# Row chunks of every fourth feature in the x blocks, and weight slices loaded by GpSimd, in a fused attention and expert kernel

## The chip, the cores and the metric

The kernel runs on one core of a Trainium2 chip. The metric is the device time of one execution in microseconds (us); lower is better. Where several executions are compared, the median is taken.

## What is computed

Three stages follow each other: attention over a window of 128 positions and four sink positions, a top-1 mixture of experts, and a feed-forward layer with a squared ReLU. All is float32. The change is in the third stage alone.

```python
def reference(**kwargs):
    attn_out = _attn_ref(**attn_kwargs)              # 4 x 8 heads, 768 positions, 64 wide
    x = attn_out.transpose(0, 2, 1, 3).reshape(3072, 512)
    x = _moe_ref(x=x, **moe_kwargs)                  # x + gate * relu(x @ w1[e]) @ w2[e], skipped rows keep x
    return _moe2_ref(x=x, **moe2_kwargs)

def _moe2_ref(x, w_in, w_out):                       # 3072 x 512, 512 x 2048, 2048 x 512
    h = x @ w_in
    r = np.maximum(h, 0.0)
    g = r * r
    return (g @ w_out).astype(np.float32)
```

## The kernel before

The first two stages leave x as rows of 512 floats in a DRAM tensor, x_rows. In the third stage each matrix product is made from two rounded parts, an upper and a lower one (upper = a copy to the rounded type by ScalarE, lower = source minus upper by VectorE), with three matmuls for one: lower weights by upper data, upper by upper, upper weights by lower data.

Both matrix products of the third stage use a Strassen-like form: the operands are split in 2 x 2 blocks, and seven products of blocks replace eight. The products are numbered 1 to 7; TensorE takes them in the order 1, 5, 6, 2, 7, 4, 3 (in step 0: 1, 2, 5, 6, 7, 4, 3). A product of the first layer is 12 matmuls of 128x512. Products 1 and 2 use plain blocks of x, products 5, 6, 7 and 4 use differences of blocks (`x_sum`), product 3 a plain one.

The first layer has three chunks of 1024 tokens (m), each with four steps that differ in the weight slice (s); so there are 12 steps t = 4m + s. In a step ScalarE copies product 1 from PSUM to q1 (`p1_copy`, line 1086) and makes block 11 (`block11`, lines 1092 and 1094), VectorE makes the three other blocks (`u2` line 1919, `u3_z22` lines 1925 and 1930, `z21` line 1941, `z12` line 1947) and squares them (line 1935), and SyncE stores four results of 512 KB in g_rows (`store_g`, line 629). The next step's `p1_copy` waits until the store of q1 has landed; product 5 waits for `z12` of the step before; product 3 waits for `u3_z22`, which follows product 7. The second layer then has three chunks of seven products of four units, 12 matmuls each (`unit`, lines 1514, 1515 and 1519), which read g_rows back; a unit's parts are made at lines 1110 and 1956.

The x blocks. SyncE loads x for chunk 1 in step 2 and for chunk 2 in step 5, in `load_x` (line 592): 8 blocks of 512 tokens by 128 features, each by four loads of 32 partitions. A run in DRAM is 32 floats, 128 bytes. VectorE turns each block in squares of 32 (`turn_later`, line 1900), two of the eight turns in step 2 and six in step 3 for chunk 1, four in step 5 and four in step 6 for chunk 2. For the second half of chunk 0 the same is done in the opening (`first_in`, `turn_first`, line 1893); the first half is turned by TensorE (line 1528). The x blocks overlie the buffer of the weight slices, so they can't be loaded while it is used.

The weight slices. Slices s = 0 and 1 of the first layer's weights are ready when it begins. `later_w` holds six more: k = 0 and 1 are slices s = 2 and 3 of the first layer, k = 2 to 5 the four slices of the second layer. Slice k is loaded into `w_in8` by two loads of 512 KB that SyncE issues (lines 584 and 585), GpSimd makes four sums of it (lines 864 to 869), ScalarE three upper parts (`slice_upper`, line 1080) and VectorE three lower parts (`slice_lower`, line 1912; semaphore s_wpl). SyncE issues them in the order of its queue: slice 0 before the opening, slice 1 in step 1, slice 2 at the begin of step 9 after the stores of step 8, slices 3 and 4 at the begin of steps 10 and 11, slice 5 in step 11. The parts of slices 2, 3 and 4 are made in steps 9, 10 and 11: on ScalarE behind `p1_copy`, on VectorE behind `u2`. All queues are in order; the order is written out by hand.

The last results of the second layer are turned by VectorE (line 1982) and stored by SyncE in `store_y` (line 668), four stores of 32 partitions for each half.

## Time and profile before

| | |
|---|---|
| time, median of 3 runs | 920.34 us (919.03 to 921.26) |
| time of the profiled execution | 921.18 us |
| its span in the profile | 919.5 us |
| TensorE busy | 853.1 us, 93% of the span |
| VectorE busy | 680.8 us, 74% |
| ScalarE busy | 454.9 us, 49% |
| GpSimd busy | 121.5 us, 13% |
| DMA moved | 155.34 MB, 99869 of 142678 packets under 512 bytes |

In the rows, PE is TensorE's matmuls, PEld its weight loads, DVE VectorE, ACT ScalarE, POOL GpSimd, SP SyncE; SPq is SyncE's queue. L1478 is line 1478 of the kernel. Times are in us from the start of the span unless they are marked otherwise. "x16" counts instructions. In a timeline the brackets hold the idle time of the engine before the instruction and what ended it. Neighbouring matmuls overlap in the timeline: from start to start a 128x512 one takes 0.227 us at the full clock. The granted clock is a share of full speed, 2.4 GHz. "DMA to landing" is the time from issue until the data is there.

### The profile page before, as it was taken

Reading aid. Unit: us, or ns where it says so; the run is one execution under the profiler, and the core shown is the slowest. Engines: PE = TensorE matmul, PEld = TensorE weight load, DVE = VectorE, ACT = ScalarE, POOL = GpSimd, SP = SyncE. Lnnn points to the kernel's source line nnn. Section 1 sums busy time; section 2 is a strip of 40 time slices with the busy share of each in tenths; the row PEclk is TensorE's granted clock in tenths of the full one; section 3 lists DMA queues with packets and bytes.
Section 4 is the critical chain, followed back from the end, with each engine's and each line's share of the span. In section 5 each row is a group of like instructions: output and inputs, shape, how many; then the busy total and the mean of one; then the engine's idle time right before and its main releaser. Section 6 shows DMA issues by size and latency. Waiting matters only on the chain.

```text
span 919.5 us, 16261 instructions
## 1 busy us (share of the span) xinstructions
PE 853.1 (93%) x4960; PEld 690.0 (75%) x4961; DVE 680.8 (74%) x1533; ACT 454.9 (49%) x900; POOL 121.5 (13%) x170
## 2 busy tenths in 40 slices
PE   9999999999999999969959999977869999999996
PEld 7778777767888887748837878766657888888885
DVE  5787899876777769667748578754479779868964
ACT  7888999855666668332214113222233434334341
POOL 3112222233211123110200000022220000000000
PEclk9999999999999999989979999989979999999999
DMA  5556665187566686332462553322474683576433
GB/s 200 173 165 211 229 224 174 70 287 272 202 225 238 246 289 227 119 68 95 137 158 92 148 151 136 121 108 92 161 274 145 175 224 115 167 198 168 137 78 61
DMA packets 142678, 155.34 MB, mean 169 GB/s; under 512 B 99869, under 2 KB 99997, under 8 KB 142608
## 3 DMA queue, kind: packets, MB, share of 16 engines
q1 hardware_dynamic: 136320, 138.65, 47.7%
q0 software_dynamic: 6000, 15.49, 4.8%
q8 instruction: 36, 0.59, 0.3%
q10 hardware_dynamic: 288, 0.34, 0.1%
q14 instruction: 34, 0.28, 0.1%
HBM read 108.13 MB, written 50.73 MB: 173 GB/s over the span
## 4 chain that ended last, share of the span: by engine, by line
PE 72%; DVE 8%; DMA 5%; issue 4%; SPq 3%; ACT 3%; POOL 2%; DVEq 1%; ACTq 0%; POOLq 0%
PE banks L1519 8%; PE banks L1514 8%; PE banks L1515 8%; PE banks L1344 8%; PE banks L1363 7%; PE banks L1478 5%; PE banks L1479 5%; PE banks L1483 5%; PE banks L1191 4%; PE banks L1246 4%; PE banks L1219 4%; DMA w_in<-in_later_w 3%; SPq L592 3%; DVE w_lo L1912 2%; PE banks L1257 1%
## 5 line engine op out<-in xcount | busy, mean ns | idle before, releaser
L1478 PE MATMUL banks<-xh,w_lo 128*128 128x512 f32 x336 | 137.5, 409 | 39.9 <-DVE q L1930 15.6
L1514 PE MATMUL banks<-xh,w_lo 128*128 128x512 f32 x336 | 132.1, 393 | 5.6 <-ACT xh L1110 5.6
L1479 PE MATMUL banks<-xh,w_hi 128*128 128x512 f32 x336 | 135.6, 404 | 0.0
L1515 PE MATMUL banks<-xh,w_hi 128*128 128x512 f32 x336 | 131.8, 392 | 0.0
L1478 PEld LDWEIGHTS banks<-xh,w_lo 128*128 128x128 f32 x336 | 66.1, 197 | 58.7 <-issue 18.9
L1483 PE MATMUL banks<-xl,w_hi 128*128 128x512 f32 x336 | 107.2, 401 | 0.0
L893 ACT ACTIVATE prob<-score,neg_max 128x264 f32<-128x264 f32 (+1 forms) x192 | 94.0, 496 | 14.0 <-DVE neg_max L1575 13.9
L1519 PE MATMUL banks<-xl,w_hi 128*128 128x512 f32 x336 | 90.0, 390 | 1.1 <-DVE xl L1956 1.1
L1838 DVE TENSOR_TENSOR w_lo<-w_raw,w_hi x70 | 81.9, 1220 | 10.3 <-ACT w_hi L1008 8.2
L1110 ACT ACTIVATE xh<-chain_g 128x1024 fp32r<-128x1024 f32 x48 | 50.8, 1060 | 71.8 <-PE banks L1519 59.6
L1575 DVE CUSTOM_DVE_ANT_0 score<-banks,masks 128x264 f32<-128x264 f32 (+1 forms) x192 | 74.1, 401 | 11.6 <-PE banks L1191 7.8
L1514 PEld LDWEIGHTS banks<-xh,w_lo 128*128 128x128 f32 x336 | 63.9, 190 | 19.3 <-issue 6.0
L1483 PEld LDWEIGHTS banks<-xl,w_hi 128*128 128x128 f32 x336 | 65.7, 196 | 14.7 <-DVE xl L1883 0.5
L1479 PEld LDWEIGHTS banks<-xh,w_hi 128*128 128x128 f32 x336 | 66.3, 197 | 13.7
L1519 PEld LDWEIGHTS banks<-xl,w_hi 128*128 128x128 f32 x336 | 63.1, 188 | 14.8 <-DVE xl L1956 1.7
L1515 PEld LDWEIGHTS banks<-xh,w_hi 128*128 128x128 f32 x336 | 63.8, 190 | 13.3
L1086 ACT ACTIVATE q<-banks 128x1024 f32<-128x1024 f32 x12 | 12.3, 1026 | 122.3 <-DMA g_rows<-q 99.5
L1008 ACT ACTIVATE w_hi<-w_raw x70 | 68.9, 1049 | 3.1 <-issue 3.1
L1956 DVE TENSOR_TENSOR xl<-chain_g,xh 128x1024 fp32r<-128x1024 f32 x48 | 58.3, 1217 | 16.0 <-ACT xh L1110 16.0
L1219 PE MATMUL banks<-ident,prob 128*128 128x128 f32 x352 | 55.3, 280 | 3.7 <-ACT probT L906 3.0
L906 ACT ACTIVATE probT<-banks 128x512 f32<-128x512 f32 (+1 forms) x96 | 53.2, 555 | 6.7 <-PE banks L1219 6.7
L1191 PE MATMUL banks<-k_in,q_in 64*128 64x264 f32 (+1 forms) x384 | 52.8, 391 | 0.3 <-DVE neg_max L1575 0.3
(194 smaller groups left out, 1641.4 us busy)
## 6 DMA issues: line engine op xcount, KB each, us to landing
w_raw<-in_weights SPq DMA_DIRECT2D x64, 512.0 KB, 5.5
g_rows<-q SPq DMA_DIRECT2D x48, 512.0 KB, 2.6
stream_g<-g_rows SPq DMA_DIRECT2D x36, 512.0 KB, 4.0
q_in<-in_qT SPq DMA_DIRECT2D x24, 256.0 KB, 3.1
v_in<-in_v SPq DMA_DIRECT2D x24, 256.0 KB, 3.5
x_rows<-x_row SPq DMA_DIRECT2D x24, 256.0 KB, 3.1
w_in<-in_later_w SPq DMA_DIRECT2D x12, 512.0 KB, 5.7
chain_g<-g_rows SPq DMA_DIRECT2D x12, 512.0 KB, 5.5
```

What stands on the lines that cost most here:

```text
L893: eng.activation(prob[:, i % 2, h, 0:width(i)], score[:, i % 2, h, 0:width(i)], ACT.Exp, bias=neg_max[:, i % 2, h:h + 1], scale=-1.0, accu ...
L1191: eng.matmul(score_ps[n % SCORE_BANKS][:, 0:width(i)], q_in[rows, i % 3, h // 2, :], keys, start=True, stop=True).then_inc(s_score, 1)
L1219: ins = eng.transpose(to[:, u * P:(u + 1) * P], prob[:, i % 2, 2 * k + half, at * KB + NS:(at + 1) * KB], ident[:, :])
L1344: ins = eng.matmul(h_ps[half][:, :], x[:, c, :], w[:, c, cols], start=(c == 0 and k == 0), stop=(c == DC - 1 and k == 2))
L1478: eng.matmul(to, w(w_lo, j, c), xh[p][:, c, :], start=(c == 0 and p in (1, 5, 6, 4)), stop=False, skip_group_check=True)
L1479: eng.matmul(to, w(w_hi, j, c), xh[p][:, c, :], start=False, stop=False, skip_group_check=True)
L1483: ins = eng.matmul(to, w(w_hi, j, c), xl[p][:, c, :], start=False, stop=(c == 1), skip_group_check=True)
L1514: eng.matmul(to[c], w(w_lo, j, c), hi[:, j, :], start=(q == 0 and j == 0 and p in (1, 5, 6, 4)), stop=False, skip_group_check=True)
L1515: eng.matmul(to[c], w(w_hi, j, c), hi[:, j, :], start=False, stop=False, skip_group_check=True)
L1519: ins = eng.matmul(to[c], w(w_hi, j, c), lo[:, j, :], start=False, stop=(q == 3 and j == 1), skip_group_check=True)
L1575: eng.tensor_tensor_reduce(score[:, i % 2, h, 0:width(i)], score_ps[n % SCORE_BANKS][:, 0:width(i)], masks[:, mask_kind(i), 0:len(blocks(i ...
L1838: eng.tensor_tensor(w_lo[1 - slot][:, f, :], w_raw[:, f, :], w_hi[1 - slot][:, f, :].bitcast(F32), ALU.subtract).then_inc(s_wlo, 1)
```

## The change

Feature blocks of x are now taken as every fourth feature (4 i + c for block c), where they were 128 neighbouring ones; the rows of w_in are permuted on the host in the same way. A load of 32 partitions so fetches runs of 128 floats, 512 bytes: 8 loads of 256 KB replace the 32 loads of 64 KB for a chunk, and 4 replace 16 in the opening, two of them issued by ScalarE. The turns and the transposes by TensorE read their input with a step of four floats. The eight turns of a chunk are four in steps 2 and 5 and four in steps 3 and 6.

GpSimd issues the loads of the weight slices itself, in the order 0, 1, 2, 4, 3, 5, each before its sums. Slice 3 is loaded into the places of its own upper and lower parts, once step 9 is over, and its parts are made there; it is loaded in four pieces. Slices 0, 1, 2 and 4 have their parts made at the begin of steps 1, 2, 9 and 11, ahead of `p1_copy` and of `u2`; slice 3 in step 10, behind `block11` on ScalarE and behind `z21` and its square on VectorE.

The last result's stores are issued half by SyncE and half by ScalarE.

```diff
+IN_PLACE = 3
...
-        x_in = [at(f"x_in{n}", [P, SUPER // BLOCK, BLOCK], F32, w_raw_at + 4 * SUPER * (n + 1) if n < 7 else blocks_at[2] + 4 * BOTH) for n in range(8)]
-        x_turned = [at(f"x_turned{n}", [P, 2, SUPER], F32, w_raw_at + n * 4 * BOTH) for n in range(4)]
-        first_in = [at(f"first_in{n}", [P, SUPER // BLOCK, BLOCK], F32, q_at[1 + n // 2] + n % 2 * 4 * SUPER) for n in range(4)]
+        x_in = [at(f"x_in{n}", [P, SUPER // BLOCK, P], F32, w_raw_at - 4 * P + 4 * SUPER * (4 * n + 1)) for n in range(2)]
+        x_turned = [at(f"x_turned{n}", [P, SUPER // BLOCK, P], F32, w_raw_at - 4 * P + n * 4 * SUPER * DC) for n in range(2)]
+        assert w_raw_at - 4 * P + 4 * SUPER * 9 <= blocks_at[0]
+        early_b12 = at("early_b12", [P, 2, SUPER], F32, q_at[2])
         w_in8 = at("w_in8", [P, 8, SUPER], F32, w_raw_at)
+        raw_hi = at("raw_hi", [P, UNIT, CH], F32, w_raw_at + 4 * UNIT * CH)
+        raw_lo = at("raw_lo", [P, UNIT, CH], F32, w_raw_at + 2 * 4 * UNIT * CH)
...
+        def by_chunk(turned, first):
+
+            return turned[:, :, first * BLOCK:(first + 2) * BLOCK].rearrange("p g (c t) -> p c g t", t=BLOCK)
+
+        def by_block(part):
+
+            return part.rearrange("p c (g t) -> p c g t", t=BLOCK)
+
+        def x_block(n):
+
+            return by_chunk(x_turned[n % 2], n // 2 * 2)
+
+        def x_source(m, p):
+
+            if m == 0:
+                return {1: by_block(pb), 2: by_block(pd), 7: by_block(early_b12[:, :, :]), 3: by_block(early_b22[:, :, :])}.get(p, by_block(early_chain[:, :, :]))
+            return x_block({1: 0, 5: 0, 6: 0, 4: 0, 7: 1, 2: 2, 3: 3}[p])
+
+        def features(row, c):
+
+            return row[:, c:DM:DC]
...
+        def raw_slice(k):
+
+            if k != IN_PLACE:
+                return [w_in8[:, n, :] for n in range(8)]
+            return [raw_hi[:, LATER[3], SUPER:CH]] + [raw_lo[:, n, SUPER:CH] for n in range(1, 8)]
+
+        def sums_place(k):
+
+            return (0, 1, 2, 4, 3, 5).index(k)
...
+        def load_x(eng, m, half, b, to, done):
+
+            first = m * BOTH + half * SUPER
+            rows = x_rows[first:first + SUPER, b * P:(b + 1) * P].rearrange("(g t) f -> t g f", t=BLOCK)
+            eng.dma_start(to[b * BLOCK:(b + 1) * BLOCK, :, :], rows).then_inc(done, 16)
...
-            load_slice(0)
             eng.wait_ge(s_bscatter, tiles * 16 + 16)
             close(eng)
             eng.wait_ge(s_cturn, 4)
-            for c in range(DC):
-                load_x(0, 1, c, first_in[c], s_cx[c])
-
-            x_order = ((0, 0), (0, 1), (1, 0), (1, 1), (0, 2), (0, 3), (1, 2), (1, 3))
+            for b in range(2):
+                load_x(eng, 0, 1, b, first_in, s_xin[2])
+
             for t in range(STEPS):
                 if t in (2, 5):
 
...
                         eng.wait_ge(s_wpl, 6)
                     else:
                         eng.wait_ge(s_xl, x_made(1, 3))
-                    for n, (token_half, c) in enumerate(x_order):
-                        load_x((t + 2) // 3, token_half, c, x_in[n], s_xin[n // 2])
-                if t == 9:
-                    eng.wait_ge(s_xl, x_made(2, 3))
-                    load_slice(2)
-                if t in (10, 11):
-                    load_slice(t - 7)
...
+                    for half in range(2):
+                        for b in range(P // BLOCK):
+                            load_x(eng, (t + 2) // 3, half, b, x_in[half], s_xin[half])
...
-                if t == 1:
-                    eng.wait_ge(s_wpl, 3)
-                    load_slice(1)
-                if t in (9, 10):
-                    eng.wait_ge(s_wpl, 3 * (t - 6))
...
-                    eng.wait_ge(s_wpl, 15)
-                    load_slice(5)
...
-            store_y(2, "z12")
+                store_y(eng, m, "z21", range(4))
+            store_y(eng, 2, "z12", (0, 1))
...
+            def load_slice(k):
+
+                raw = raw_slice(k)
+                for places, part in ((slice(0, 2), slice(0, 2)), (slice(4, 7, 2), slice(2, 4))):
+                    if k == IN_PLACE and places.start == 0:
+                        eng.dma_start(raw[0], later_w[k, :, 0, :]).then_inc(s_win, 16)
+                        eng.dma_start(raw[1], later_w[k, :, 1, :]).then_inc(s_win, 16)
+                    elif k == IN_PLACE:
+                        eng.dma_start(raw[4], later_w[k, :, 2, :]).then_inc(s_win, 16)
+                        eng.dma_start(raw[6], later_w[k, :, 3, :]).then_inc(s_win, 16)
+                    else:
+                        eng.dma_start(w_in8[:, places, :], later_w[k, :, part, :]).then_inc(s_win, 16)
+
             def weight_sums(k):
 
-                eng.wait_ge(s_win, 32 * k + 32)
-                a21, a11, s1, s2, a12, s3, a22, s4 = (w_in8[:, n, :] for n in range(8))
+                eng.wait_ge(s_win, 32 * sums_place(k) + 32 + 32 * (sums_place(k) >= sums_place(IN_PLACE)))
+                a21, a11, s1, s2, a12, s3, a22, s4 = raw_slice(k)
                 eng.tensor_tensor(s1, a21, a22, ALU.add).then_inc(s_wsum, 1)
                 eng.tensor_tensor(s3, a11, a21, ALU.subtract).then_inc(s_wsum, 1)
-                eng.wait_ge(s_wsum, 4 * k + 1)
+                eng.wait_ge(s_wsum, 4 * sums_place(k) + 1)
                 eng.tensor_tensor(s2, s1, a11, ALU.subtract).then_inc(s_wsum, 1)
-                eng.wait_ge(s_wsum, 4 * k + 3)
+                eng.wait_ge(s_wsum, 4 * sums_place(k) + 3)
                 eng.tensor_tensor(s4, a12, s2, ALU.subtract).then_inc(s_wsum, 1)
 
-            for k in range(6):
-                weight_sums(k)
+            load_slice(0)
+            weight_sums(0)
+            eng.wait_ge(s_wpl, 3)
+            load_slice(1)
+            weight_sums(1)
+            eng.wait_ge(s_xl, x_made(2, 3))
+            load_slice(2)
+            weight_sums(2)
+            eng.wait_ge(s_wpl, 9)
+            load_slice(4)
+            weight_sums(4)
+            eng.wait_ge(s_one, halves(9, 3))
+            load_slice(3)
+            weight_sums(3)
+            eng.wait_ge(s_wpl, 15)
+            load_slice(5)
+            weight_sums(5)
...
+            x_upper(0, 2)
             eng.wait_ge(s_bscatter, tiles * 16 + 16)
             close(eng)
+            for b in range(2, 4):
+                load_x(eng, 0, 1, b, first_in, s_xin[2])
             for t in range(STEPS):
+                if t in (1, 2, 9, 11):
+                    for piece in range(3):
+                        slice_upper({1: 0, 2: 1, 9: 2, 11: 4}[t], piece)
                 p1_copy(t)
                 if t == 0:
                     block11(0)
                     for p in (5, 6, 7, 4, 3):
-                        x_upper(0, p, x_source(0, p))
+                        x_upper(0, p)
                 if t in (3, 7):
-                    x_upper((t + 1) // 4, 1, x_source(1, 1))
-                    x_upper((t + 1) // 4, 5, x_source(1, 5))
+                    x_upper((t + 1) // 4, 1)
+                    x_upper((t + 1) // 4, 5)
                 if t in (4, 8):
-                    x_upper(t // 4, 4, x_source(1, 4))
-                    x_upper(t // 4, 3, x_source(1, 3))
-                if t in (1, 2, 9, 10, 11):
-                    for piece in range(3):
-                        slice_upper({1: 0, 2: 1, 9: 2, 10: 3, 11: 4}[t], piece)
+                    x_upper(t // 4, 4)
+                    x_upper(t // 4, 3)
                 if t == STEPS - 1:
                     unit_upper(0, 1, 0)
...
+                if t == 10:
+                    for piece in range(3):
+                        slice_upper(3, piece)
...
+            store_y(eng, 2, "z12", (2, 3))
...
-                    eng.matmul(xT0_ps[c][:, n * P:(n + 1) * P], x_c[:, n, c * P:(c + 1) * P], ident[:, :], is_transpose=True,
+                    eng.matmul(xT0_ps[c][:, n * P:(n + 1) * P], features(x_c[:, n, :], c), ident[:, :], is_transpose=True,
...
             def turn_first(c):
 
-                eng.wait_ge(s_cx[c], 16 + 16 * (P // BLOCK))
+                if c == 0:
+                    eng.wait_ge(s_xin[2], 16 * (P // BLOCK))
                 to = (early_b12, early_b22)[c // 2]
-                eng.transpose(to[:, c % 2, :], first_in[c][:, :, :].rearrange("p g f -> p (g f)")).then_inc(s_xturn, 1)
-
-            def turn_later(m, n):
-
-                eng.wait_ge(s_xin[n // 2], 32 * (P // BLOCK) * m)
-                if n > 0:
-                    turned_to(8 * m - 4 + n)
-                eng.transpose(x_turned[n // 2][:, n % 2, :], x_in[n][:, :, :].rearrange("p g f -> p (g f)")).then_inc(s_xturn, 1)
+                eng.transpose(to[:, c % 2, :].rearrange("p (g t) -> p g t", t=BLOCK), first_in[:, :, c:P:DC]).then_inc(s_xturn, 1)
+
+            def turn_later(m, half, n):
+
+                eng.wait_ge(s_xin[half], 16 * (P // BLOCK) * m)
+                if half + n > 0:
+                    turned_to(8 * m - 4 + 4 * half + n)
+                part = slice(n * DC, n * DC + DC)
+                eng.transpose(x_turned[half][:, part, :].rearrange("p g (c t) -> p g c t", t=BLOCK),
+                              x_in[half][:, part, :].rearrange("p g (f c) -> p g c f", f=BLOCK)).then_inc(s_xturn, 1)
...
+            turn_first(0)
+            turn_first(1)
             turned_to(2)
-            x_sum(chain_x, b12_x, pb)
-            x_lower(0, 5, chain_x)
+            x_sum(chain_0, b12_0, by_block(pb))
+            x_lower(0, 5)
+            turn_first(2)
+            turn_first(3)
             turned_to(4)
...
                 if t in (3, 6):
-                    for n in range(2 if t == 3 else 4, 8):
-                        turn_later((t + 2) // 3 if t == 6 else 1, n)
+                    for n in range(4):
+                        turn_later(t // 3, 1, n)
                 if t in (3, 7):
-                    turned_to(4 + 8 * (m + 1) - 0)
-                    x_lower(m + 1, 1, xt[0])
-                    x_sum(xt[0], xt[1], xt[0])
+                    turned_to(8 * (m + 1) + 4)
+                    x_lower(m + 1, 1)
+                    x_sum(b11_x, b12_x, b11_x)
                 if t in (4, 8):
-                    x_lower(m, 2, xt[2])
-                    x_lower(m, 7, xt[1])
+                    x_lower(m, 2)
+                    x_lower(m, 7)
+                if t in (1, 2, 9, 11):
+                    for piece in range(3):
+                        slice_lower({1: 0, 2: 1, 9: 2, 11: 4}[t], piece)
                 u2(t)
...
-                if t in (1, 2, 9, 10, 11):
-                    for piece in range(3):
-                        slice_lower({1: 0, 2: 1, 9: 2, 10: 3, 11: 4}[t], piece)
...
                 relu_square(q1, (s_z21, t + 1), s_g21)
+                if t == 10:
+                    for piece in range(3):
+                        slice_lower(3, piece)
...
                 if t in (2, 5):
-                    for n in range(2 if t == 2 else 4):
-                        turn_later(1 if t == 2 else 2, n)
+                    for n in range(4):
+                        turn_later((t + 1) // 3, 0, n)
...
-    w_in = moe2_w_in.reshape(2, 2, P, 2, QUARTERS, 2, P).transpose(4, 2, 3, 0, 5, 1, 6).reshape(QUARTERS, P, 4, SUPER)
+    w_in = moe2_w_in.reshape(P, DC, DFF).transpose(1, 0, 2).reshape(2, 2, P, 2, QUARTERS, 2, P).transpose(4, 2, 3, 0, 5, 1, 6).reshape(QUARTERS, P, 4, SUPER)
```

## Rows read from the trace of the kernel before

**Rows 1.** Stretches: us, length, busy us per engine (count), granted clock, DMA share, GB/s.

```profile
459.00:493.00 34.00, 22.69 (x91) 18.06 (x90) 21.65 (x25) 7.96 (x8) 0.00 (x0) 0.85 0.54 140
...
592.00:700.00 108.00, 85.81 (x330) 68.44 (x329) 62.40 (x58) 31.97 (x31) 20.35 (x16) 0.87 0.46 166
...
700.00:911.00 211.00, 211.00 (x932) 174.71 (x932) 169.38 (x156) 81.79 (x78) 0.00 (x0) 1.00 0.53 147
```

**Rows 2.** TensorE's waits, 388 to 700 us: releaser, us in total, times, longest.

```profile
PE banks L1478 <- DVE q L1930: 15.6, 3, 5.3
...
PE banks L1514 <- ACT xh L1110: 5.6, 1, 5.6
```

**Rows 3.** Timeline of TensorE: start us, us, line, operation, count, idle before, releaser.

```profile
403.25 0.80 PE L1478 MATMUL banks<-xh,w_lo 128*128 128x512 f32 x1 [5.48 <-ACT xh L1064]
...
462.62 0.47 PE L1478 MATMUL banks<-xh,w_lo 128*128 128x512 f32 x1 [0.72 <-DVE q L1947]
...
478.89 0.77 PE L1478 MATMUL banks<-xh,w_lo 128*128 128x512 f32 x1 [10.59 <-ACT q L1086]
...
496.42 0.47 PE L1478 MATMUL banks<-xh,w_lo 128*128 128x512 f32 x1 [1.70 <-DVE q L1947]
...
536.43 0.50 PE L1478 MATMUL banks<-xh,w_lo 128*128 128x512 f32 x1 [1.65 <-DVE q L1947]
...
613.85 0.80 PE L1478 MATMUL banks<-xh,w_lo 128*128 128x512 f32 x1 [5.21 <-DVE q L1930]
...
620.08 0.40 PE L1479 MATMUL banks<-xh,w_hi 128*128 128x512 f32 x1
...
695.33 1.20 PE L1519 MATMUL banks<-xl,w_hi 128*128 128x512 f32 x4 [1.07 <-DVE xl L1956]
```

**Rows 4.** Timeline of SyncE's DMA issues.

```profile
390.28 8.30 SPq L592 DMA_DIRECT2D first_in<-x_rows  x16
...
453.52 18.56 SPq L592 DMA_DIRECT2D x_in<-x_rows  x32
...
595.23 0.43 SPq L584 DMA_DIRECT2D w_in<-in_later_w  x1
...
913.50 4.10 SPq L668 DMA_DIRECT2D out<-y_b  x8
```

**Rows 5.** Timelines of GpSimd, ScalarE and VectorE in step 9: one slice.

```profile
601.59 1.28 POOL L864 TENSOR_TENSOR w_in<-w_in 128x512 f32<-128x512 f32 x1 [154.54 <-DMA w_in<-in_later_w]
...
606.83 3.38 ACT L1080 ACTIVATE w_hi<-w_in 128x1024 fp32r<-128x1024 f32 x3 [10.65 <-POOL w_in L869]
...
607.92 4.08 DVE L1912 TENSOR_TENSOR w_lo<-w_in,w_hi 128x1024 fp32r<-128x1024 f32 x3 [6.18 <-ACT w_hi L1080]
```

**Rows 6.** Stretches, the first of 128-byte packets, the second of 2 KB packets.

```profile
454.00:473.00 19.00, 13.58 (x59) 10.62 (x57) 12.07 (x15) 0.00 (x0) 0.00 (x0) 1.00 0.70 109
...
596.00:601.00 5.00, 5.00 (x24) 4.13 (x22) 0.48 (x1) 0.18 (x1) 0.00 (x0) 1.00 0.90 288
```

**Rows 7.** VectorE: four turns, the last x parts of chunk 2, a lower unit.

```profile
532.11 3.16 DVE L1900 STREAM_TRANSPOSE x_turned<-x_in 128x512 f32<-128x512 f32 x4
...
582.62 2.35 DVE L1883 TENSOR_TENSOR xl<-x_turned,xh 128x1024 fp32r<-128x1024 f32 x2
...
687.84 1.22 DVE L1956 TENSOR_TENSOR xl<-chain_g,xh 128x1024 fp32r<-128x1024 f32 x1
```

**Rows 8.** Slice loads by SyncE; loads of x_raw by GpSimd and by SyncE.

```profile
DMA to landing us min/median/max: 5.4/5.8/8.1
...
L831 POOL DMA_DIRECT2D x_raw<-routed x14: 541/553/577, 205.9 to 363.6; - x14
...
DMA to landing us min/median/max: 3.0/6.2/7.0
...
x_raw<-routed SPq DMA_DIRECT2D x2, 260.0 KB, 2.7
```

**Rows 9.** Weight loads of the transposes at line 1528.

```profile
L1528 PEld LDWEIGHTS banks<-ident,x_row x16: 138/140/143, 385.3 to 387.1; 128*128 128x128 f32 x16
```

115 lines of the change are left out of this document (52 added, 63 removed).

## The prediction

> **What bounds the kernel now.** I read the table of the profile first: TensorE is busy 93% of the span, so the change can only be worth TensorE's idle and slow stretches. The stretches [rows 1] show where they lie. From 700 to 911 us TensorE is busy without a gap at granted clock 1.00; from 459 to 493 it is busy 22.7 of 34 us at 0.85, and from 592 to 700 it is busy 85.8 of 108 us at 0.87. The waits [rows 2] name who is late most: VectorE's sums at line 1930 (15.6 us in three waits) and ScalarE's parts at line 1110. The single waits [rows 3] give places. I call the twelve steps of the second network's first layer 0 to 11; a product is 12 matmuls of 0.227 us, 2.72 us, and a step of seven is 19.04 us. In step 0 product 5 starts 5.48 us late; in step 3 product 2 starts 10.59 us late; in steps 9, 10 and 11 product 3 starts 5.2 us late on the mean. After each such pause 15 matmuls take 6.23 us (613.85 to 620.08) where 3.40 is normal: 2.8 us more, at the lower granted clock (1.2 of 2.4 GHz).
>
> Causes, from the queues [rows 4]. In step 2 SyncE issues 32 loads of x blocks, 18.56 us, ahead of the stores of that step; ScalarE may not overwrite q1 until its store is done, so product 2 of step 3 waits. In steps 9 to 11 SyncE asks for a slice only after the step before has stored; the pair of loads, GpSimd's four sums from 601.59 on, ScalarE's three upper parts (606.83, 3.38 us) and VectorE's three lower parts (4.08 us) run in a row [rows 5], and VectorE's sums of product 7 stand behind the lower parts.
>
> **Part 1: x blocks of 512-byte runs.** 32 loads of 64 KB become 8 of 256 KB, with the same 32 partitions x 16 pieces in each. I price an issue as before, 18.56/32 = 0.58 us, so 4.6 us. For the packets [rows 6]: at 128 bytes, 0.70 x 16 x 19 us for 109 GB/s x 19 us is 13 ns each; at 2 KB, 0.90 x 16 x 5 us for 288 GB/s x 5 us is 102 ns. A line between gives an estimate of 31 ns for 512 bytes, so 4096 of them take 7.9 us on 16 engines (bounds: 3.4 us if a packet costs 13 ns whatever it holds, 13.5 us if the rate stays that of 128 bytes). SyncE starts when the lower parts of slice 1 are made. These move to the begin of step 2 (440.1 us, 19.04 before product 1 of step 3 at 459.2): slice 0's lowers can end near 428, four operations after VectorE's last of step 0, and with the 12.65 us of part 2 for load and sums GpSimd's sums of slice 1 end about 441, uppers 444.6, lowers 446.4. The blocks are down near 456, before VectorE reaches the turns at 459.5. The 10.6 us wait and its 2.8 us of slow clock go.
>
> What is late next: VectorE. Four turns take 3.16 us [rows 7] and stand before the sum for which product 5 of the next step waits. Step 6 has that pattern today: 1.65 us [rows 3]. So step 3 pays 1.65. From that sum on, in us after the step's start and in operations of 1.2 us: sum 4.4, square 5.5, four other turns 8.6, two for the new chunk 10.9, product 6's sum 12.1, three for the chunk 15.5, product 7's four half sums 18.0, square, product 4's sum and square 21.6, two for the chunk 23.9, last sum 25.1. Nothing of TensorE's waits in between (product 7 wants 12.5, product 3 wants 18.0), but product 5 of step 4 wants the last sum at 23.4: 1.7 us more (it is 1.70 today, at 496.42). Steps 3 and 4 pay 3.4 us; today it is 0.72 + 10.59 + 1.70 + 2.8 = 15.8. **Gain 12.5 us.** Steps 5 to 8 keep their order and 1 to 2 us waits: nothing.
>
> Opening: 16 loads issued over 8.30 us [rows 4] become two on SyncE and two on ScalarE (about 1 us of ScalarE before it is needed). Each block is complete only when all four are, and GpSimd's slice 0, 1 MB, now goes out at 388.6 instead of 382, right ahead. 2 MB together need about 8 us, so the first sum starts near 401.1 instead of 400.9 to 402.1, and product 5 starts 0 to 1 us sooner than 403.25. I take 0.5 (bounds -3 and +4). Slice 0's parts hide in step 0, where ScalarE idles after 411.
>
> **Part 2: slices loaded by GpSimd, parts at a step's begin.** I call L the time from GpSimd's first issue until both loads of a slice are down. SyncE's pair took 6.3 us (595.23 to 601.59). No slice went through GpSimd, but x_raw of 260 KB did: landing 6.2 us [rows 8], against 2.7 us for the two that SyncE issued. Bounds of L: 6.3 and 6.3 + 3.5 = 9.8; I take 7.5, nearer to the slice's own row, since GpSimd's issue is 0.55 us whatever VectorE does. Four sums are 5.15 us.
>
> Times on the old axis, as if steps 0 to 8 took as long as now. Step 9 starts at 592.4. The last x part of chunk 2 is made by 585.0 [rows 7]; load and sums of slice 2 end at 585.0 + 7.5 + 5.15 = 597.7, uppers 601.1, ScalarE's copy of product 1 at 602.1; product 2 wants it at 592.4 + 8.16 = 600.5: **1.6 us** late (0 to 3.9 by L). Lowers end at 602.9, and VectorE's sums of product 7 are free again: the three waits at line 1930 go, with their slow clock. Slice 4: 602.9 + 12.65 = 615.5. Slice 3, four loads, in place: 615.5 + 8.1 + 5.15 = 628.8. Step 10 starts at 613.0; uppers of slice 3 632.2. Its lowers stand on VectorE before the last sum: 632.1 (19.1 into the step) + 4.08 + 1.2 = 637.4, where product 5 of step 11 wants it at 613.0 + 21.76 = 634.8: a **new wait of 2.6 us**. Step 11 ends at 613.0 + 38.08 + 2.6 = 653.7. Lowers of slice 4 end at 642.7. Slice 5 meets the loads of g; today its second load takes 8.1 us where the median is 5.8 [rows 8], 2.3 more: 642.7 + 7.5 + 2.3 + 5.15 = 657.7, uppers 661.1, upper unit 662.1, lower unit 663.3. From the end of that lower unit (689.1) to TensorE's restart at 695.33 today VectorE does one slice part, three sums and one more lower unit, 6.3 us [rows 3, 7]; so the restart comes at 669.6. TensorE by itself would be there at 653.7 + 10.9 + 1.8 = 666.4. 695.3 - 669.6: **gain 25.7 us**. After that nothing changes: 216 us to the last matmul with no gap.
>
> **Part 3: tail.** The last 8 stores are 4.10 us on SyncE [rows 4]; halved over two queues, 2.05. **Gain 2.0** (0 to 2.3).
>
> **Reads with a step of four elements.** The 20 turns, and the 24 weight loads of the opening's transposes, read every fourth float. No row shows such a read. Turns now 0.79 us, loads 0.14 us [rows 7, 9]. I take nothing, the nearest rows being the same instructions with packed reads; upper bound twice: below.
>
> Two rules of the Trainium skill speak against the change. "Advanced Engine Details and Errata", Memory Cachelines, says that SBUF is read in lines of 16 bytes and that a different line for each access costs; every fourth float is just that, and rival A prices it. "SBUF — State Buffer", SBUF: two separate sides, says that a DMA issued by GpSimd can wait for its descriptors while VectorE holds the port they share; the trace's plain issues of 541 to 577 ns next to a busy VectorE speak against it, and rivals B and D are what it would do.
>
> **Sum.** 0.5 + 12.5 + 25.7 + 2.0 = 40.7 us. The profiled execution took 921.18 us (span 919.5), 0.84 above the median of 920.34: 921.18 - 40.7 - 0.8 = 879.7, so 880.
>
> **Rivals.**
> A. Turns cost double: 3.2 us for each four. The last sums of steps 2 and 5 come 3.2 us later each, step 3's chain about 2.6, the opening 2 (weight loads included): 11 us, 891. For it: nothing here reads so. Against it: a turn of 512 elements at 0.71 us is no faster than any other operation.
> B. GpSimd's loads are slow but not ruinous, L = 9.8 to 11. Load, sums, uppers, lowers follow each other four times, so TensorE's restart comes at 636.6 + 4L on the old axis: 675.8 to 680.6, 6 to 11 us later: 886 to 891, with slow clock after the pauses up to 895. For it: 6.2 us for half a slice's load. Against it: those loads ran among 256 GB/s of weights.
> C. The x blocks are no faster: issues that cost four times 0.58 us, or 512-byte packets at the old rate. The loads then still begin 7 us sooner (446.6, not 453.5), SyncE is free at 465.2 and not at 472.1, and the copy of product 1 of step 3 is in time; the second half of the blocks lands near 467.5, product 6's sum comes 2.5 us late, and with the same in step 6: 3 to 5 us, 884. Against it: 128-byte packets moved 109 GB/s at 0.70 busy, 2 KB packets 288 at 0.90.
> D. Slower than before: the same chain as B, starved, with no bottom. The restart is 14.9 us (the other gains) past 695.3, at 710.2, when 636.6 + 4L says L = 18.4 us. From there on the kernel is slower; at L = 20 it takes 927. Against it: the slowest GpSimd load of x_raw is far from that (maximum 7.0).
>
> **How the numbers follow.** Forecast 0.52, with a range of its own from 874 to 886; A 0.19; B 0.17; C 0.06; D 0.04; 0.02 for another loss about as large as the gain, of which 0.01 ends as slower. Leaving out D and the far ends of A to C together gives 873 to 896. A measurement of this kernel tells no change from 0.2%, 1.8 us: faster 0.94, same 0.01, slower 0.05.
>
> **What would show it.** SyncE's x loads 8 times in about 5 us, then no 10 us wait in step 3; product 5 of steps 3 and 4 under 2 us late. No wait at VectorE's product 7 sums in steps 9 to 11, a new one of 2 to 3 us in step 11 for the last sum, and from 1 to 2 us in step 9 for ScalarE's copy. GpSimd's loads down 7 to 8 us after issue. Turns at 0.71 us. TensorE's granted clock above 0.95 where it was 0.87. The forecast is wrong if any of these takes a wait over 4 us, above all L over 9 us or turns over 1 us.

## The result and the profile after

The changed kernel takes 897.9 us (median of 4 runs, 896.67 to 898.67) where the kernel before takes 920.44 (919.03 to 921.26) beside it: a ratio of 0.9755, interval 0.9738 to 0.9773. It is 22.5 us faster; the prediction had 40.7 us and a time of 880, with a range up to 896. The profiled execution took 897.29 us (span 895.8), against 921.18 (919.5).

I call "stage 3" the stretch from TensorE's first product of step 0 (390.19 us before, 390.40 after) to VectorE's last sum (911.51 before, 888.85 after). It went from 521.3 to 498.5 us. The rest of the kernel ahead of it is untouched, and its length differs by a few us from run to run, so I compare kernels by the length of stage 3 in their profiled executions, and the whole time by ratios.

The head of the page after:

```profile
PE 848.1 (95%) x4960; PEld 686.2 (77%) x4961; DVE 689.8 (77%) x1533; ACT 455.3 (51%) x900; POOL 130.3 (15%) x184
...
DMA packets 110262, 155.34 MB, mean 173 GB/s; under 512 B 57981, under 2 KB 68349, under 8 KB 110192
```

TensorE's busy time fell by 5 us with the same matmuls: less time at the lower clock. VectorE's rose by 9 us, though it does the same operations; its 20 turns, 0.37 us longer each, are 7.4 of that. The stretches that answer to [rows 1] (same columns):

```profile
461.00:506.00 45.00, 40.06 (x170) 32.41 (x170) 40.45 (x41) 12.98 (x13) 0.00 (x0) 0.96 0.25 102
588.00:673.00 85.00, 75.03 (x311) 59.71 (x310) 59.98 (x55) 30.53 (x29) 27.72 (x24) 0.96 0.53 195
673.00:889.00 216.00, 215.81 (x952) 178.33 (x951) 173.71 (x160) 83.45 (x79) 0.00 (x0) 1.00 0.52 148
```

The granted clock is 0.96 where it was 0.85 and 0.87, and the last 216 us are as gapless as before. TensorE's waits from 388 to 700 us, which answer to [rows 2]:

```profile
PE banks L1527 <- DVE q L2000: 11.6, 5, 3.2
PE banks L1527 <- ACT xh L1112: 7.4, 3, 6.1
PE banks L1527 <- ACT q L1129: 4.1, 2, 2.9
PE banks L1568 <- DVE xl L2009: 4.0, 3, 3.2
PE banks L1527 <- DVE q L1972: 2.0, 2, 1.4
```

VectorE's product 7 sums (15.6 us, the first row of [rows 2]) are gone from the list; what leads now is VectorE's last sum of a step (L2000), five times. The single waits, as in [rows 3]:

```profile
404.10 0.80 PE L1527 MATMUL banks<-xh,w_lo 128*128 128x512 f32 x1 [6.11 <-ACT xh L1112]
...
466.91 0.76 PE L1527 MATMUL banks<-xh,w_lo 128*128 128x512 f32 x1 [3.21 <-DVE q L2000]
...
489.29 0.47 PE L1527 MATMUL banks<-xh,w_lo 128*128 128x512 f32 x1 [1.73 <-DVE q L2000]
...
530.75 0.50 PE L1527 MATMUL banks<-xh,w_lo 128*128 128x512 f32 x1 [3.12 <-DVE q L2000]
...
599.30 0.71 PE L1527 MATMUL banks<-xh,w_lo 128*128 128x512 f32 x1 [2.87 <-ACT q L1129]
...
637.31 0.80 PE L1527 MATMUL banks<-xh,w_lo 128*128 128x512 f32 x1 [2.54 <-DVE q L2000]
...
672.73 1.20 PE L1568 MATMUL banks<-xl,w_hi 128*128 128x512 f32 x4 [3.15 <-DVE xl L2009]
```

The same instruction can be found in both traces, so the gain can be read off along the way (before, after, gained so far, forecast):

| TensorE's instruction | before | after | gained | forecast |
|---|---|---|---|---|
| step 0, product 7 (the 1.41 us wait) | 412.65 | 414.49 | -1.8 | 0.5 |
| step 4, product 5 | 496.42 | 489.29 | 7.1 | 13.0 |
| step 6, product 5 | 536.43 | 530.75 | 5.7 | 13.0 |
| step 8, product 5 | 575.75 | 571.70 | 4.1 | 13.0 |
| restart in the second layer | 695.33 | 672.73 | 22.6 | 38.7 |
| last sum of stage 3 (VectorE) | 911.51 | 888.85 | 22.7 | 38.7 |
| end of the execution | 921.18 | 897.29 | 23.9 | 40.7 |

So 9.0 us are missing by step 8, 7.1 between there and the restart, and 1.0 in the tail. This is VectorE in step 2, around the turns; first as it is after, then the row of the turns over the whole kernel (min/median/max ns):

```profile
459.88 1.23 DVE L1988 SCALAR_TENSOR_TENSOR q<-q 128x1024 f32<-128x1024 f32 x1
461.02 4.64 DVE L1951 STREAM_TRANSPOSE x_turned<-x_in 128x512 f32<-128x512 f32 x4
465.59 1.17 DVE L2000 TENSOR_TENSOR q<-q,banks 128x1024 f32<-128x1024 f32 x1
...
L1951 DVE STREAM_TRANSPOSE x_turned<-x_in x16: 1078/1084/1103, 461.0 to 535.5; 128x512 f32<-128x512 f32 x16
```

Four turns take 4.64 us where they took 3.16 [rows 7], with no other work in between. The sum that product 5 waits for is late by just that.

### The profile page after: what moved, and what is told of

It reads as the page before. It is cut to its first block, busy times and chain, and to the rows that moved or that the text cites. A ratio compares the mean times of both kernels' runs of the same rounds, so it can differ in the third digit from the quotient of the medians.

```text
span 895.8 us, 16201 instructions
## 1 busy us (share of the span) xinstructions
PE 848.1 (95%) x4960; PEld 686.2 (77%) x4961; DVE 689.8 (77%) x1533; ACT 455.3 (51%) x900; POOL 130.3 (15%) x184
## 4 chain that ended last, share of the span: by engine, by line
PE 74%; DVE 12%; issue 6%; DMA 4%; ACT 2%; POOL 1%; DVEq 0%; ACTq 0%; POOLq 0%; SPq 0%
PE banks L1568 8%; PE banks L1563 8%; PE banks L1564 8%; PE banks L1393 8%; PE banks L1412 7%; PE banks L1527 5%; PE banks L1528 5%; PE banks L1532 5%; PE banks L1240 5%; PE banks L1295 4%; PE banks L1268 4%; PE banks L1306 1%; PE banks L1401 1%; DVE x_turned L1951 1%; DVE xl L1932 1%
## 5 line engine op out<-in xcount | busy, mean ns | idle before, releaser
L1527 PE MATMUL banks<-xh,w_lo 128*128 128x512 f32 x336 | 135.8, 404 | 25.0 <-DVE q L2000 11.6
L1528 PE MATMUL banks<-xh,w_hi 128*128 128x512 f32 x336 | 134.0, 399 | 0.0
L1563 PE MATMUL banks<-xh,w_lo 128*128 128x512 f32 x336 | 130.7, 389 | 0.0
L1564 PE MATMUL banks<-xh,w_hi 128*128 128x512 f32 x336 | 130.7, 389 | 0.0
L1528 PEld LDWEIGHTS banks<-xh,w_hi 128*128 128x128 f32 x336 | 65.3, 194 | 13.4
L1564 PEld LDWEIGHTS banks<-xh,w_hi 128*128 128x128 f32 x336 | 63.0, 188 | 13.1
L1412 PE MATMUL banks<-w_lo,hb_hi 128*128 128x512 f32 x120 | 50.0, 417 | 0.0
```

What stands on the lines that cost most here:

```text
L1412: ins = eng.matmul(y_ps[:, :], h[:, c // 4, at], w[:, DC + c // 2, cols], start=(c == 0 and k == 0), stop=(c == FC - 1 and k == 2))
L1527: eng.matmul(to, w(w_lo, j, c), xh[p][:, c, :], start=(c == 0 and p in (1, 5, 6, 4)), stop=False, skip_group_check=True)
L1528: eng.matmul(to, w(w_hi, j, c), xh[p][:, c, :], start=False, stop=False, skip_group_check=True)
L1563: eng.matmul(to[c], w(w_lo, j, c), hi[:, j, :], start=(q == 0 and j == 0 and p in (1, 5, 6, 4)), stop=False, skip_group_check=True)
L1564: eng.matmul(to[c], w(w_hi, j, c), hi[:, j, :], start=False, stop=False, skip_group_check=True)
```

## The experiments

All times are medians of 4 runs with the ratio against the kernel before on the same chip (921.85, 920.66 and 921.61 us on the three chips used). The changed kernel's ratio is 0.9755 and its stage 3 is 498.5 us. The length of stage 3 is from one profiled execution each, and so is "to the restart": from TensorE's first product of step 0 to its restart in the second layer, 282.3 us in the changed kernel. Both depend on how much low clock followed the waits in that one execution (the last section has the spread), so differences of 1 to 2 us between two kernels can be chance.

### 1. The turns read packed floats

The x blocks load as in the change, but VectorE's 20 turns read 32 neighbouring floats each. The features of a chunk then come out in the wrong order, so this kernel computes other numbers; instructions, transfers and waits are the same.

```diff
-first_in[:, :, c:P:DC])
+first_in[:, :, c * BLOCK:(c + 1) * BLOCK])
...
-x_in[half][:, part, :].rearrange("p g (f c) -> p g c f", f=BLOCK)
+x_in[half][:, part, :].rearrange("p g (c f) -> p g c f", f=BLOCK)
```

> The changed kernel, but VectorE's 20 turns read 32 neighbouring floats instead of every fourth one (the features of the x blocks are so mixed up: this changes what is computed, not how much). Theory (the step of four floats makes a turn 1.16 us where it was 0.79): turns take 0.79 us again; the waits for the last sum in steps 3 and 6 shrink from 3.2 and 3.1 us to about 1.7 and lose the 1.4 to 1.7 us of low clock behind them, and the opening gains about 1.4: 7 us in all, 891. Rival (the turns are slower because of their destination's pattern or the place they stand in): turns stay at 1.16 us and the time at 898.

Measured: 890.28 us, ratio 0.9658 (0.9637 to 0.9678), stage 3 494.0 us. The turns, and TensorE's waits in steps 3 and 6:

```profile
L1951 DVE STREAM_TRANSPOSE x_turned<-x_in x16: 704/711/712, 458.1 to 526.9; 128x512 f32<-128x512 f32 x16
...
462.50 0.47 PE L1527 MATMUL banks<-xh,w_lo 128*128 128x512 f32 x1 [1.74 <-DVE q L2000]
...
523.33 0.50 PE L1527 MATMUL banks<-xh,w_lo 128*128 128x512 f32 x1 [1.65 <-DVE q L2000]
```

The step of four floats costs 0.37 us a turn. Without it the waits are 1.74 and 1.65 instead of 3.21 and 3.12, the forecast's own 1.65. The ratios differ by 0.0097, 8.9 us (6.4 to 11.4 by the two intervals); to the restart it is 276.4 instead of 282.3 us, 6 us less. The two waits and the opening (5.56 + 0.17 us of waits for 6.11 + 0.67) are 4.0 of that; the rest is the clock, below. The clock also took something back: behind the wait of step 9 this execution lost 3.0 us to it where the changed kernel's lost 1.7, and behind the restart 1.6 where the changed kernel's lost 0.1, which is why stage 3 as a whole shows only 4.5.

### 2 and 3. Each part alone

Kernel 2 has the x blocks and the tail of the change, while SyncE loads the slices at the old places and their parts stand where they stood. Kernel 3 is the kernel before with the slices' part alone. The core of the edit (2 takes it away from the changed kernel, 3 adds it to the kernel before):

```diff
 GpSimd:
-for k in range(6):
-    weight_sums(k)
+load_slice(k); weight_sums(k)   for k in 0, 1, 2, 4, 3, 5
 SyncE:
-load_slice(0) ... load_slice(5)
 ScalarE and VectorE:
+slice parts ahead of p1_copy(t) and u2(t), in steps 1, 2, 9, 11
-slice parts at the end of steps 1, 2, 9, 10, 11
```

> Only the x blocks and the tail are changed; the weight slices are loaded by SyncE and have their parts made in the old places. Theory (the two parts depend on each other, since the x loads can only begin when slice 1's lower parts are made): the x loads begin at 453 us and not at 448, are down near 463, and turns of 1.16 us follow; step 3 then waits about 7 us in place of 10.6 and the gain is small: 917. Rival (the parts add up): the gain before step 9, 4.3 us, and 1.1 of the tail are kept: 915. Second rival (the 512-byte runs alone take the wait of step 3 away, as predicted): 908 or less.

Measured: 914.28 us, ratio 0.9931 (0.9906 to 0.9956), stage 3 513.7 us. SyncE's queue, and the waits at VectorE's last sum in steps 3, 4 and 6; the wait of 10.59 us for q1 is gone:

```profile
453.06 5.36 SPq L438 DMA_DIRECT2D x_in<-x_rows  x8
...
465.88 0.77 PE L1514 MATMUL banks<-xh,w_lo 128*128 128x512 f32 x1 [4.44 <-DVE q L1987]
...
488.38 0.47 PE L1514 MATMUL banks<-xh,w_lo 128*128 128x512 f32 x1 [0.96 <-DVE q L1987]
...
529.86 0.50 PE L1514 MATMUL banks<-xh,w_lo 128*128 128x512 f32 x1 [3.13 <-DVE q L1987]
```

> The kernel before with only the weight slices changed: loaded by GpSimd, slice 3 in place, parts at a step's begin; the x blocks keep their 128-byte runs and packed turns. Theory: from step 9 to the restart in the second layer it gains the same 18 us as the whole change, and since slice 1's lower parts come 5 us sooner, so do the x loads, and step 3 waits about 6 us instead of 10.6: 897, so that the new x blocks bring next to nothing. Rival (the x blocks are worth what the trace shows before step 9): 902.

Measured: 901.32 us, ratio 0.9766 (0.9734 to 0.9797), stage 3 501.1 us. SyncE's queue, the opening's wait, step 3's and step 4's:

```profile
449.91 17.59 SPq L600 DMA_DIRECT2D x_in<-x_rows  x32
...
406.10 0.79 PE L1506 MATMUL banks<-xh,w_lo 128*128 128x512 f32 x1 [8.39 <-ACT xh L1087]
...
474.51 0.47 PE L1506 MATMUL banks<-xh,w_lo 128*128 128x512 f32 x1 [4.03 <-ACT q L1111]
...
492.04 0.47 PE L1506 MATMUL banks<-xh,w_lo 128*128 128x512 f32 x1 [1.81 <-DVE q L1976]
```

The x blocks alone bring 7.6 us, the slices alone 20.5 (by the ratios 6.4 and 21.6); together 28, more than the 22.5 of both. The two overlap in steps 0 to 4, because each of them alone takes away most of step 3's wait. From product 7 of step 0 to product 5 of step 4 the kernel before takes 83.8 us, kernel 2 76.2, kernel 3 76.6 and the changed kernel 74.8: 7.6 and 7.1 us for either part, 9.0 for both. In kernel 2 SyncE is free after 5.4 us of issues. In kernel 3 the 32 old loads still keep it for 17.6 us, but they begin at 449.9, not 453.5, since slice 1's parts are earlier, and they are over at 467.5, not 472.1; the rest of the change from 10.59 to 4.03 us is mostly that TensorE itself comes later, after a longer wait in the opening. In the opening it is the other way round: GpSimd's 1 MB beside 16 loads of 128-byte runs makes the wait 8.39 us, and the blocks' 512-byte runs bring it back to 6.11. What the blocks bring on top of the slices is 2 us by the medians, 1 by the ratios and 4.1 by the profiled executions, of which 1.4 is the tail (8.33 us after the last sum in kernel 3, 6.95 in the changed kernel).

### 4. Slice 3's lower parts behind the last sum

```diff
-if t == 10: slice_lower(3, piece) x3     # behind z21 and its square
 z12(t)
 relu_square(q2, ...)
+if t == 10: slice_lower(3, piece) x3
```

> The changed kernel with slice 3's three lower parts made behind the last sum and its square of step 10, not ahead of them. Theory (the wait of 2.5 us in step 11 and the 1.5 us of low clock behind it come from that place alone): product 5 of step 11 waits under 0.5 us, product 7's sum comes about 1 us late instead, and the kernel gains 3 us: 895. Rival (VectorE bounds the passage into the second layer anyway, from its own queue): the restart there stays where it is and the time stays within 1 us of 898.

Measured: 898.08 us, ratio 0.9749 (0.9733 to 0.9766), stage 3 497.5 us. The 2.54 us wait of step 11 is gone (one of 0.71 us at another sum takes its place), but the restart still waits 3.20 us for VectorE. To the restart this execution takes 2.6 us less, so the rival's "stays where it is" doesn't hold there; behind the restart it loses 1.6 us to the lower clock that the changed kernel's didn't, and by the ratios the two kernels can't be told apart (0.6 us).

### 5. Slice 2's parts behind ScalarE's copy and `u2` in step 9

```diff
-if t in (1, 2, 9, 11): slice parts        # ahead of p1_copy(t) / u2(t)
+if t in (1, 2, 11): slice parts
 p1_copy(t)                                # on VectorE: u2(t)
+if t == 9: slice parts of slice 2
```

> The changed kernel with step 9 in the old order: slice 2's upper parts behind the copy of product 1 on ScalarE, its lower parts behind product 6's sum on VectorE; the slice is still loaded by GpSimd ahead of the step. Theory (the wait of 2.9 us for ScalarE's copy in step 9 exists because the parts at the step's begin stand before it while the slice's sums end 7 us into the step): no wait in step 9, nor the 1.5 us of low clock behind it, 4 us less: 0.9955 of the changed kernel, 894. Rival (the parts then come late for product 7's sums, as in the kernel before): a wait of 2 us or more at those sums, no gain.

Measured: 897.13 us, ratio 0.9716 (0.9671 to 0.9761), stage 3 497.1 us. The wait of 2.87 us is gone and step 11's grew from 2.54 to 5.25: the slice's places come free later, so slices 4 and 3 are asked for 1.0 and 2.2 us later after the start of stage 3, and VectorE idles 2.34 us for slice 3's upper parts ahead of the last sum. Neither forecast fits: the rival's wait at product 7's sums doesn't come, and to the restart the kernel takes 3.0 us less. By the ratios it is 3.6 us, with an interval from 0.8 us more to 8.0 less: unclear.

### 6. Chunk 2's turns spread in steps 5 and 6

```diff
-if t == 5: turn_later(2, 0, n) x4        # ahead of the last sum
 z12(t)
 relu_square(q2, ...)
+if t == 5: turn_later(2, 0, n) x4
 ...
-if t == 6: turn_later(2, 1, n) x4        # in one piece
+if t == 6: turn_later(2, 1, n) x2 ahead of product 6's sum, x2 behind the last sum
```

> The changed kernel with chunk 2's turns moved: four behind the last sum and square of step 5, two behind product 6's sum of step 6, two behind the last square of step 6. Theory (a turn costs time only where it stands before a sum that TensorE waits for): the 3.1 us wait of step 6 and its 1.7 us of low clock go, and nothing comes instead: 4.8 us less, 893. Rival (VectorE has no room there, so the wait appears at product 6's or 7's sums): under 2 us gained.

Measured: 891.84 us, ratio 0.9670 (0.9623 to 0.9716), stage 3 494.8 us. Step 6 has no wait any more, and to the restart it takes 5.1 us less, where the wait itself was 3.12: the clock is most of the rest (1.75). By the ratios it is 7.8 us (3.3 to 12.4).

### 7 and 9. The passage into the second layer

Both let VectorE make lower units of the second layer between its own sums there, in place of all sums first. Kernel 7 moves each unit to the place right behind its sum; kernel 9 keeps the sums one or two ahead of the units.

```diff
-t1(0, q) for all q, then unit_lower / t2 / unit_lower / t3 in turns
+7: t1(0, q); unit_lower(0, 5, q) ...; t2(0, 0); t2(0, 1); unit_lower(0, 6, 0) ...
+9: t1(0, 1); unit_lower(0, 5, 0); t1(0, 2); unit_lower(0, 5, 1); t1(0, 3); unit_lower(0, 5, 2); t2(0, 0); ...
```

> The changed kernel, in which VectorE makes the lower part of product 5's first unit in the second layer ahead of three sums that it doesn't need, and takes the sums in between the units that follow. Theory (VectorE's own queue from product 4's end in step 11 sets the restart, not the last slice's load): the 3.15 us wait goes and at most 0.5 us comes instead later: 3 us less, 895. Rival (the last slice's load and sums bound the passage, as I predicted): the wait stays, 898.

Measured: 901.06 us, ratio 0.9768 (0.9722 to 0.9815), stage 3 504.3 us: by the ratios no better than the changed kernel, by stage 3 5.8 us worse. The 3.15 us wait is gone, so the wait was VectorE's order of work and not the last slice's load, and the units then come every 3.55 us, where TensorE needs 2.72:

```profile
671.38 0.47 PE L1563 MATMUL banks<-xh,w_lo 128*128 128x512 f32 x1 [1.18 <-ACT xh L1153]
...
674.93 0.47 PE L1563 MATMUL banks<-xh,w_lo 128*128 128x512 f32 x1 [0.56 <-ACT xh L1153]
...
678.47 0.47 PE L1563 MATMUL banks<-xh,w_lo 128*128 128x512 f32 x1 [0.57 <-ACT xh L1153]
```

Sum on VectorE, upper unit on ScalarE, lower unit on VectorE ran one after the other, for every unit.

> The changed kernel with the sums at the passage into the second layer interleaved otherwise: each lower part now stands two operations behind the sum whose upper part it needs, so that ScalarE's 1.1 us lies beside another VectorE operation (in the first try it lay between them and a unit took 3.5 us). Theory (VectorE's queue sets the restart): the wait of 3.15 us falls to about 0.9 and no unit waits more than 0.3 us behind it; 2 us less, from TensorE's first product to its last. Rival (what is taken out at the restart comes back when the fourth block's stream is loaded late): a wait of about 2 us at product 2, no gain.

Measured: 895.03 us, ratio 0.9706 (0.9676 to 0.9736), stage 3 498.0 us. The restart waits 0.91 us, with 1.31 and 0.72 ahead of it. By the ratios 4.5 us (1.3 to 7.7), by stage 3 0.5: how much it brings by itself stays open between these.

### 8 and 10. Slice 0 later in the opening

```diff
+eng.wait_ge(s_xin[2], 16 * (P // BLOCK))   # GpSimd: the opening's x blocks are down
 load_slice(0)
+eng.wait_ge(s_xsum, 4)                     # kernel 10 only
 weight_sums(0)
```

> The changed kernel, in which GpSimd waits with slice 0's load until the x blocks of the opening are down. Theory (the two share the DMA engines; the kernel with only the x blocks changed, where SyncE had loaded slice 0 earlier, started product 5 2.3 us sooner): the wait before product 5 of step 0 falls from 6.1 to about 4 us, slice 0's parts still hide in step 0: 2 us less, 896. Rival (the load of 512-byte packets is what takes that long): nothing.

Measured: 901.78 us, ratio 0.9765 (0.9719 to 0.9811), stage 3 501.4 us. Product 5 of step 0 starts 3 us earlier, and all is given back. GpSimd, and VectorE beside it:

```profile
406.26 1.29 POOL L895 TENSOR_TENSOR w_in<-w_in 128x512 f32<-128x512 f32 x1 [5.41 <-DMA w_in<-in_later_w]
407.51 2.25 POOL L896 TENSOR_TENSOR w_in<-w_in 128x512 f32<-128x512 f32 x1
409.73 2.24 POOL L898 TENSOR_TENSOR w_in<-w_in 128x512 f32<-128x512 f32 x1
412.05 2.15 POOL L900 TENSOR_TENSOR w_in<-w_in 128x512 f32<-128x512 f32 x1
...
407.03 1.60 DVE L1937 TENSOR_TENSOR early_chain<-early_b,early_chain 128x1024 f32<-128x1024 f32 x1
408.55 2.29 DVE L1937 TENSOR_TENSOR early_b<-early_b,early_b 128x1024 f32<-128x1024 f32 x1
410.77 2.29 DVE L1933 TENSOR_TENSOR xl<-early_chain,xh 128x1024 fp32r<-128x1024 f32 x1
```

Operations of 1.28 and 1.22 us take 2.2 to 2.3 on both engines, and TensorE waits 2.14 us for that xl.

> The changed kernel; GpSimd loads slice 0 when the opening's x blocks are down, and makes its sums when VectorE's four sums of x are made. Theory (the first try gained 2.9 us at product 5 and lost more to GpSimd's and VectorE's sums standing in each other's way, 2.25 and 2.29 us each in place of 1.28 and 1.22): sums of 1.2 us on both, product 7 of step 0 starts about 2.3 us sooner than in the changed kernel, 2.3 us less in all. Rival (VectorE's operations are slowed by slice 0's transfer, not by GpSimd's sums): they stay at 1.6 to 2.3 us and nothing is gained.

Measured: 894.33 us, ratio 0.9711 (0.9684 to 0.9739), stage 3 495.5 us. GpSimd's sums begin at 410.4, behind VectorE's urgent operations, which take 1.22 us again; the opening's wait is 4.65 us instead of 6.11. GpSimd's own sums still take 2.2 to 2.4 us there, not the 1.2 of the theory, but nothing waits for them. Product 7 of step 0 comes 1.5 us sooner after the start of stage 3. The rest of the 3.0 us is low clock that didn't follow step 6's wait of 3.13 us in this execution.

### 11 and 12. The orders together

Kernel 11 has the orders of 4, 5, 6, 9 and 10. Kernel 12 also spreads chunk 1's turns, as 6 does for chunk 2:

```diff
-if t == 2: turn_later(1, 0, n) x4        # ahead of the last sum
+if t == 2: turn_later(1, 0, n) x2 there, x2 behind the last sum
-if t == 3: turn_later(1, 1, n) x4, then chunk 1's parts and sums
+if t == 3: turn_later(1, 1, n) x2 there, x2 behind u2(t); parts and sums in between, three behind the last sum
```

> The changed kernel with five orders of work changed at once: slice 3's lower parts behind the last square, step 9 in the old order, chunk 2's turns moved, the passage interleaved, slice 0 later. Theory (each wait of 2.5 to 3.2 us costs itself and 1.4 to 1.8 us of low clock, and all of them are matters of place in VectorE's and ScalarE's queues): 2.6 + 3.5 + 4.8 + 2 + 2.3 = 15 us from first product to last, less 2 for what they share: 885. Rival (VectorE is so full in this stage that waits only move): 891, as the best one alone.

Measured: 882.05 us, ratio 0.9588 (0.9541 to 0.9635), stage 3 484.6 us: the theory's outcome (885), not the rival's.

> The kernel with all five orders, and chunk 1's turns spread as well: two before the last sum of step 2, four behind its square, two behind product 6's sum of step 3, with the chunk's sums and parts between VectorE's other work. Theory: step 3 waits 0.9 us and not 3.2 plus 1.4 to 3.0 of low clock, step 4 about 1.7 us: 4 us less than with the five orders alone, 881. Rival (in steps 3 and 4 VectorE has about as much work as there is time, so that what leaves one wait enters the next): within 1 us of the five orders.

Measured: 878.23 us, ratio 0.9532 (0.9506 to 0.9558), stage 3 479.6 us. The stretches of kernel 12 (columns as in [rows 1]), then its waits:

```profile
388.00:430.00 42.00, 34.33 (x133) 26.08 (x133) 32.72 (x29) 14.65 (x14) 10.58 (x8) 0.92 0.35 109
430.00:585.00 155.00, 151.51 (x665) 124.13 (x664) 123.89 (x120) 42.81 (x42) 13.28 (x10) 1.00 0.46 148
585.00:666.00 81.00, 77.28 (x334) 62.04 (x333) 69.00 (x62) 34.18 (x33) 25.80 (x20) 1.00 0.54 195
...
PE banks L1532 <- ACT xh L1114: 4.9, 2, 4.2
PE banks L1532 <- DVE q L2005: 3.5, 3, 1.7
```

Behind the opening no wait is over 1.7 us and the clock is 1.00. The orders add up and don't help each other: to the restart kernels 4, 5, 6, 9 and 10 take 2.6, 3.0, 5.1, 1.7 and 3.0 us less than the changed kernel, 15.4 in all, and kernel 11 with all of them 15.1. By the ratios the five give 20.5 us in all and kernel 11 15.4. Over the whole of stage 3 it looks different, 9.4 us for the five and 13.9 together, because of the low clock behind the restart: kernels 4, 5 and 6 lost 1.6 to 1.8 us to it, the changed kernel's one execution 0.1. Kernel 12 beats both kernels, by 43 us against the kernel before (4.7%), and the turns in it still read with a step of four.

## Why the prediction was wrong

The direction and the main mechanisms were right and the gain was mis-sized, 40.7 for 22.5 us. Two terms that the sum had at nothing are the larger part of it: the strided reads, and the slow clock behind the waits that stay or come. Of the 17.1 us that the table misses, 4.4 are the longer turns (3.0 in steps 3 and 6, 1.4 in the opening), 6.4 the low clock (3.2 of it behind the two waits that the turns made longer), 1.8 the waits of steps 9 and 10, 1.7 the passage, 1.0 the tail, and the rest the opening and a charge of the sum that was too high. By its own steps:

**"Reads with a step of four elements": "I take nothing".** This is the step that failed. A turn takes 1.08 us for 0.71, and four in a row 4.64 for 3.16 [rows 7]: 1.5 times, half the price that rival A had put on it ("turns cost double"). The prediction had named turns over 1 us as a sign that it is wrong. The waits of steps 3 and 6 are 1.5 us longer each, by the 1.48 us that four turns take more. Experiment 1 takes away only this and gets 6 us (to the restart) or 8.9 us (by the ratios, 6.4 to 11.4) back. Rival A's time of 891 lies closer to the result than the forecast. The Trainium skill, "Advanced Engine Details and Errata", section Memory Cachelines, said that a new 16-byte line for each access has a price; the trace agrees, and I gave the rule too small a chance since no row had a size for it. The other reads with such a step, TensorE's 16 weight loads in the opening (the prediction counted 24), grew too, and the matmuls that they feed are longer than they are (283 ns, before 273), so I count them as hidden:

```profile
L1577 PEld LDWEIGHTS banks<-ident,x_row x16: 198/209/212, 385.4 to 387.3; 128*128 128x128 f32 x16
L1577 PE MATMUL banks<-ident,x_row x16: 272/283/285, 385.6 to 387.4; 128*128 128x128 f32 x16
```

**Slow clock behind a wait.** This is the second step that failed. The prediction charged it to the waits that go (2.8 us each) and nothing to those that stay or come, not even to the wait of 2.6 us that it forecast itself. Four stretches of 3 us of the changed kernel, behind the waits of 3.21, 1.73, 3.12 and 2.54 us:

```profile
466.90:469.90 3.00, 2.99 (x8) 2.37 (x9) 2.90 (x3) 0.37 (x1) 0.00 (x0) 0.53 0.35 145
489.30:492.30 3.00, 3.00 (x13) 2.51 (x14) 3.00 (x3) 2.07 (x3) 0.00 (x0) 1.00 0.36 146
530.70:533.70 3.00, 2.95 (x8) 2.35 (x9) 2.86 (x3) 0.00 (x0) 0.00 (x0) 0.57 0.31 126
637.30:640.30 3.00, 2.99 (x7) 2.42 (x8) 3.00 (x3) 0.00 (x0) 0.00 (x0) 0.50 0.32 130
```

At 0.53, 0.57 and 0.50 TensorE is at the lower of its two levels (1.2 GHz) for most of the stretch, and does 7 or 8 matmuls where 13 fit. From the starts of the matmuls, against 0.227 us each, that is 1.41, 1.75 and 1.55 us, and 1.71 behind the wait of 2.87: 6.4 us that no term of the sum held. The shorter wait costs 0.1. So 1.5 us more of turns turned waits of 1.65 us, which cost little more than their own length, into waits of 3.2, which cost 1.4 and 1.75 more on top. That is why experiments 1 and 6 gave back more than the waits they took away.

**Part 1, gain 12.5.** SyncE's 8 loads take 5.39 us (4.6 forecast) and the blocks are down in time, so the mechanism held: no wait for q1 in step 3. But experiments 2 and 3 show that either part does most of this without the other (7.6 and 7.1 of 9.0 us): the 10.6 us wait depended on the number of the loads and on the time at which they begin. The working of part 1 has both, the fewer loads and the earlier slice, but didn't see that one would nearly do; rival C came close to it. Behind it, step 3 has 3.21 and step 4 1.73 us (1.65 and 1.7 forecast). And "Steps 5 to 8 keep their order and 1 to 2 us waits: nothing" was wrong by 3.2 us in step 6, for both reasons above. Missing by step 8: 2.3 (opening) + 1.6 + 1.4 (step 3) + 1.5 + 1.75 (step 6) = 8.5 of 9.0 us. The rest is about what the sum had charged too much: 2.8 us of slow clock behind the 10.59 us wait, where the starts of the matmuls of the kernel before show 2.1.

**Opening, gain 0.5 (bounds -3 and +4).** It lost 1.8 us. GpSimd's slice 0 and the blocks load together as said; VectorE's first two turns start at 399.65 and each takes 0.37 us more, two more stand ahead of the next sum, and a second wait (0.67) comes with them. With packed turns (experiment 1) product 7 of step 0 comes 1.4 us sooner, so the turns are most of this loss.

**Part 2, gain 25.7.** It was 18.6 by the table. L came out as 7.5 us for slice 2, exactly the value taken, and between 5.4 and 9.2 for the others (slice 3's four loads 9.2, forecast 8.1; slice 5's 6.1, forecast 9.8): rivals B and D are refuted, and GpSimd's issues stay at 0.54 to 0.74 us; those of slice 2 too, where VectorE is busy for 0.9 of the time until they are down:

```profile
581.22 1.27 POOL L889 DMA_DIRECT2D w_in<-in_later_w  x2 [140.07 <-DVE xl L1932]
588.73 1.29 POOL L895 TENSOR_TENSOR w_in<-w_in 128x512 f32<-128x512 f32 x1 [6.25 <-DMA w_in<-in_later_w]
589.98 2.27 POOL L896 TENSOR_TENSOR w_in<-w_in 128x512 f32<-128x512 f32 x1
```

Slice 2's pair is also the slowest: 7.5 us, where those of slices 1 and 4, with VectorE busy for under 0.3 of the time, took 5.5 and 5.4. No run tells VectorE's part in that from that of the other transfers.

The wait of step 11 was forecast as 2.6 us for the last sum, and is 2.54, at that sum. The wait of step 9 is 2.87 instead of 1.6: one of GpSimd's four sums took 2.27 us (third row above) beside VectorE. With the clock behind both waits (3.3) and a wait of 0.55 in step 10 these are 5.1 of the 7.1 us. Most of the rest is the passage into the second layer: from its first matmul to the restart it takes 17.6 us, where the forecast has 15.9 (653.7 to 669.6). The 6.3 us from one lower unit to the restart held (666.47 to 672.73), but that lower unit itself came late, as VectorE is busy without a gap from 650.6 on. TensorE was ready 3.15 us before it. The forecast has a wait of 3.2 there (669.6 against 666.4), but for the last slice; slice 5 was down sooner than forecast and what TensorE waited for was VectorE's queue, so that this agreement is luck. I had read the passage from the trace of before, where slice 5 was late, and taken its last 6.3 us; the queue ahead of them was never written out.

**Part 3, gain 2.0 (0 to 2.3).** It was 1.0: the stage's end to the end of the span went from 7.99 to 6.95 us. ScalarE issues four of the stores in 2.10 us as forecast. But with eight stores from two queues at once each takes longer to land, on either queue: 2.2 to 2.9 us after issue for ScalarE's and 2.0 to 2.8 for SyncE's, where SyncE's last eight before took 1.7 to 1.9.

**Rival C** (blocks no faster) fell: experiment 2 shows 5.36 us where the 32 loads took 18.56. My estimate of 31 ns for a 512-byte packet was low; worked out in the same way for the stretch in which most of them move (1.04 x 16 x 9.2 us for 200 GB/s x 9.2 us) it is 43 ns, an estimate again, and inside the bounds given.

```profile
448.80:458.00 9.20, 9.20 (x42) 7.64 (x41) 4.30 (x6) 2.09 (x2) 0.00 (x0) 1.00 1.04 200
```

What stays open: how much of the 8.9 us of experiment 1 the turns bring by themselves and how much the clock, which differs from run to run (see below); and whether a layout exists that has both 512-byte runs and packed turns with the right numbers. It wasn't tried, since TensorE's transposes of the opening would need their features in runs of 32.

## What to carry to other kernels

Write out the queue of the busiest helper engine operation by operation through each stretch that the change touches, and price a wait on TensorE as its length plus, for those of 2.5 to 3.7 us here, another 1.5 us or so of matmuls at the lower clock: 1.5 us more on VectorE cost 3 us here. When a layout buys wider DMA runs with strided reads on an engine, put a price on the reads before anything else. And where several parts of a change speed up the same wait, test each alone: 7.6 and 20.5 us made 22.5. A single profiled execution can hide or invent 1.5 us per wait by its clock; compare kernels up to the same instruction as well, and check against the ratios.

## What the hardware showed that I had not expected

- **A turn of 128x512 floats takes 1.08 us when it reads every fourth float and 0.71 when it reads 32 neighbours** (16 instructions each, spread 25 and 10 ns). A weight load of 128x128 takes 209 ns for 140 in the same case.
- **The lower clock behind a pause isn't fixed by the pause's length.** The same wait of step 3, 3.2 us long at the same place in the program, is followed by a granted clock of 0.53 in the changed kernel (above) and by the first of these in kernel 7; the second is behind the restart's wait of 3.15 us in the changed kernel itself:

```profile
465.30:468.30 3.00, 2.95 (x13) 2.51 (x14) 2.90 (x3) 0.23 (x1) 0.00 (x0) 1.00 0.35 141
```

```profile
672.70:675.70 3.00, 2.97 (x13) 2.48 (x14) 2.83 (x3) 1.06 (x1) 0.00 (x0) 1.00 0.78 309
```

Over all kernels here, waits up to 1.85 us that didn't stand close behind a longer one were followed by no stretch of low clock (mostly 0.1 to 0.2 us of extra time), waits of 2.1 to 3.7 us mostly by 1.4 to 1.8 us (from 0.08 to 3.0), and waits above 4 us by 1.6 to 3.4.

- **Sums of GpSimd and two-input operations of VectorE hold each other up**: 1.28 to 2.25 us and 1.22 to 2.29 us (experiment 8). The Trainium skill, "SBUF — State Buffer", section SBUF: two separate sides, has the two engines share a pair of ports that one instruction takes whole while the other waits; the trace agrees, each operation being longer by 1.0 to 1.1 us, somewhat less than the other's length. The one sum of 2.27 us among GpSimd's sums of slice 2, which looks like such a collision, is 1.0 of the 1.3 us by which the wait of step 9 missed its forecast.
